# A linear-attention and two-MLP kernel: another order of its instructions, and eleven identity products on PE before the first keys

## What is computed

```python
def _attn_ref(q, k, v, alpha):            # (4, 8, 768, 48) each
    state = zeros(B, H, D, D)
    for t in range(S):
        state = alpha[:, :, t, :, None] * state + einsum('bhd,bhe->bhde', k[:, :, t], v[:, :, t])
        y[:, :, t] = einsum('bhd,bhde->bhe', q[:, :, t], state)

def _moe_ref(x, w_in, w_out):             # x: 3072 x 384, w_in: 384 x 2048
    h = x @ w_in
    return (h * cos(h)) @ w_out           # 3072 x 384

def _moe2_ref(x, w1, w2, w3, w_out):      # w1, w2, w3: 384 x 768
    return maximum(maximum(x @ w1, x @ w2), x @ w3) @ w_out
```

## Time and profile before

| | before |
|---|---|
| median of three runs | 859.32 us (858.6 to 860.63) |
| the profiled execution | 859.26 us |
| its span, first to last instruction | 857.6 us |
| PE busy | 825.7 us (96%), 5446 instructions |
| DVE, ACT, POOL busy | 584.3, 429.8, 232.2 us |
| granted TensorE clock, mean | 0.996 |
| DMA | 54.48 MB, mean 64 GB/s |

### The profile page before, as it was taken

The page is one execution under the profiler, slowest core; times in us unless marked ns, Lnnn a source line. Parts: engine busy times, 40 slices in busy tenths (PEclk is TensorE's granted clock), DMA queues, the critical chain, the costliest instruction groups (busy, mean ns, idle before and its releaser), DMA issues.

```text
span 857.6 us, 15503 instructions
## 1 busy us (share of the span) xinstructions
PE 825.7 (96%) x5446; PEld 759.4 (89%) x5446; DVE 584.3 (68%) x1082; ACT 429.8 (50%) x933; POOL 232.2 (27%) x262
## 2 busy tenths in 40 slices
PE   4788999999999999999999999999999999999998
PEld 4688999888888888888888878889999999999998
DVE  7778777777677767777675467767565565656454
ACT  4876776444544454444544357645343434334333
POOL 6855654433243322334233223300000000000000
PEclk9999999999999999999999999999999999999999
DMA  9742242421132223222203001310101010100001
GB/s 250 222 129 57 62 107 56 112 58 53 40 94 56 56 56 93 56 56 56 73 23 136 1 38 56 111 56 1 38 39 37 38 38 37 37 5 32 1 38 37
DMA packets 13778, 54.48 MB, mean 64 GB/s; under 512 B 1968, under 2 KB 2480, under 8 KB 13712
## 3 DMA queue, kind: packets, MB, share of 16 engines
q1 hardware_dynamic: 12992, 49.70, 20.1%
q0 software_dynamic: 720, 3.93, 1.1%
HBM read 44.19 MB, written 9.44 MB: 63 GB/s over the span
## 4 chain that ended last, share of the span: by engine, by line
PE 84%; issue 5%; POOL 4%; DVE 3%; ACT 2%; DMA 0%; DVEq 0%; POOLq 0%; ACTq 0%
PE h_ps L1264 6%; PE h_ps L1266 5%; PE h_ps L1265 5%; PE acc_pair L1264 4%; PE acc_pair L1265 4%; PE acc_pair L1266 4%; PE h_ps L1368 4%; PE score L1368 4%; PE h_ps L1370 4%; PE h_ps L1369 4%; PE score L1370 4%; PE score L1369 4%; PE acc_last L1264 2%; PE acc_last L1266 2%; PE acc_last L1265 2%
## 5 line engine op out<-in xcount | busy, mean ns | idle before, releaser
L454 POOL TENSOR_TENSOR work<-work 128x512 f32<-128x512 f32 (+1 forms) x91 | 108.1, 1188 | 297.5 <-DVE work L974 278.5
L617 ACT ACTIVATE work<-work 128x512 f32<-128x512 f32 (+1 forms) x112 | 63.7, 569 | 138.0 <-POOL work L454 120.2
L1264 PE MATMUL h_ps<-x_hi,w_hi 128*128 128x512 f32 (+1 forms) x282 | 111.5, 395 | 2.9 <-DVE work L960 1.5
L960 DVE TENSOR_TENSOR work<-work,h_ps 128x512 f32<-128x512 f32 (+1 forms) x94 | 58.7, 624 | 79.5 <-ACT work L617 79.1
L1266 PE MATMUL h_ps<-x_lo,w_hi 128*128 128x512 f32 (+1 forms) x282 | 104.2, 369 | 0.0
L1265 PE MATMUL h_ps<-x_hi,w_lo 128*128 128x512 f32 (+1 forms) x282 | 103.5, 367 | 0.0
L849 DVE RECIPROCAL inv_decay<-decay 112x128 f32<-112x128 f32 x96 | 89.4, 940 | 1.3 <-DMA raw<-qka 1.1
L1264 PE MATMUL acc_pair<-g_hi,w_hi 128*128 128x512 f32 (+1 forms) x224 | 82.1, 367 | 3.1 <-POOL g_lo L462 2.7
L624 ACT ACTIVATE g_hi<-work 128x512 fp32r<-128x512 f32 (+1 forms) x112 | 63.4, 566 | 43.1 <-DVE work L960 41.4
L1265 PE MATMUL acc_pair<-g_hi,w_lo 128*128 128x512 f32 (+1 forms) x224 | 81.0, 362 | 0.0
L1266 PE MATMUL acc_pair<-g_lo,w_hi 128*128 128x512 f32 (+1 forms) x224 | 80.9, 361 | 0.0
(11 more groups left out here) (224 smaller groups left out, 2402.4 us busy)
## 6 DMA issues: line engine op xcount, KB each, us to landing
v_all<-val SPq DMA_DIRECT2D x24, 576.0 KB, 3.7
raw<-qka SPq DMA_DIRECT2D x46, 291.0 KB, 4.8
block_out<-x SPq DMA_DIRECT2D x6, 768.0 KB, 5.9
x_in<-block_out SPq DMA_DIRECT2D x6, 768.0 KB, 4.3
raw<-wb SPq DMA_DIRECT2D x12, 384.0 KB, 3.0
out<-raw POOLq DMA_DIRECT2D x5, 768.0 KB, 3.5
stage_own<-wa SPq DMA_DIRECT2D x6, 384.0 KB, 5.7
x<-wa SPq DMA_DIRECT2D x6, 384.0 KB, 5.9
```

Source lines behind the costliest of these rows:

```text
L454: nc.gpsimd.tensor_tensor(frac[:, cols], turns[:, cols], whole[:, cols], ALU.subtract).then_inc(S["frac_done"], 1)
L617: nc.scalar.activation(cosine[:, cols], frac[:, cols], ACT.Sin, scale=-TURN if half and t < POOL_FRAC else TURN).then_inc(S["cos_done"], 1)
L960: nc.vector.tensor_tensor(gated[:, cols], cosine[:, cols], h, ALU.mult).then_inc(S["g_done"], 1)
L1264: mm(ps, w_hi[:, w_at], xh, start=first, stop=False, skip_group_check=shared)
```

## The change

No product, transfer or sum of the result is added or left out; only the eleven identity products are new, and their output is overwritten by the first outputs. What moves:

- PE: `WARM` = 11 products `ident` x `ident` into y_ps, between the wait for ident and that for k_split's zeroes. Of units 0 to 7, the score products of 4 and 5 come after the outputs of 0 and 1 (before: after 3), those of 6 and 7 after the output of 4.
- DVE, start: the wait for queries and keys comes after the first two reciprocals. The four reciprocals of group 1 come in one piece behind mask 1.
- DVE, first half of chunk 0: scans one tile earlier (in 2, 7 and 12 and ahead of the gate); the low weights of tiles 8 to 15 in tiles 5 to 11 and 13, one in each.
- DVE, chunks 1 to 4: mask and new state come ahead of the gate in row steps 1 and 2 (before: in 1 alone), and the scan comes behind whole_turns.
- POOL: group 1's keys ahead of all low weights; `mul_inverse(0, 2)` behind g_low(0); `mul_decay` and `mul_inverse` of the next groups ahead of g_low of tiles 4, 8 and 6, 12 (before: behind 4, 9 and 7, 12); low weights 5 to 7 behind g_low of tiles 0 to 2.
- ACT: another order of first_state, split_first and weight copies before the loop; the copies of the weights come two tiles later in the loop.

```diff
--- before.py
+++ after.py
@@ -42,6 +42,7 @@
 D_LO, D_HI = slice(0, HALF), slice(HALF + 2, CHUNK + 2)
 DW = CHUNK + 4
 RAWW = 2 * TOK + BATCH * DW
+WARM = 11
 QUAD = 32
 POOL_FRAC = TILES1
 XHI = PAIRS - 1 + KT
@@ -467,22 +468,22 @@
             masks()
             mul_decay(0, 1)
             mul_inverse(0, 1, slice(0, 2), "qk_half1")
-            low_weights(0)
             mul_inverse(0, 1, slice(2, BATCH))
-            low_weights(1)
-            low_weights(2)
+            for k in range(3):
+                low_weights(k)
             mul_decay(0, 2)
             low_weights(3)
             low_weights(4)
-            mul_inverse(0, 2)
             for i in range(TILES1):
+                if i in (4, 8):
+                    mul_decay(*{4: (0, 3), 8: (1, 0)}[i])
+                if i in (6, 12):
+                    mul_inverse(*{6: (0, 3), 12: (1, 0)}[i])
                 g_low(i)
-                if i in (0, 2, 3):
-                    low_weights({0: 5, 2: 6, 3: 7}[i])
-                if i in (4, 9):
-                    mul_decay(*{4: (0, 3), 9: (1, 0)}[i])
-                if i in (7, 12):
-                    mul_inverse(*{7: (0, 3), 12: (1, 0)}[i])
+                if i == 0:
+                    mul_inverse(0, 2)
+                if i < 3:
+                    low_weights(5 + i)
 
             def step(c, s, attend, prepare_next, half):
                 for i in range(TILES1):
@@ -630,21 +631,19 @@
             act.wait_ge(S["init_pool"], 6)
             first_state(0)
             first_state(1)
-            high_weights(2)
             split_first(1, 0)
+            split_first(1, 1)
             x_high0(0)
             first_state(2)
-            split_first(1, 1)
             first_state(3)
+            high_weights(2)
             first_state(4)
+            first_state(5)
+            x_high0(1)
+            first_state(6)
             high_weights(3)
-            first_state(5)
-            first_state(6)
-            x_high0(1)
+            first_state(7)
             high_weights(4)
-            first_state(7)
-            high_weights(5)
-            high_weights(6)
 
             for i in range(TILES1):
                 last = i == TILES1 - 1
@@ -661,8 +660,8 @@
                 if i in (2, 8, 14):
                     split_keys(*{2: (0, 2), 8: (0, 3), 14: (1, 0)}[i])
                 cosines(i, True)
-                if 7 + i < TILES1:
-                    high_weights(7 + i)
+                if 5 + i < TILES1:
+                    high_weights(5 + i)
             g_high(TILES1 - 1, True)
             first_state(UNITS - 1)
 
@@ -919,11 +918,11 @@
                                         ALU.subtract).then_inc(S["wlo_done"], 1)
 
             scan(0, 0)
-            dve.wait_ge(S["qka_in0"], 32)
             for part in range(2):
                 for b in range(2):
                     inverse(0, 0, 2 * part + b, 0)
                 dve.wait_ge(S["inv_done"], 2 * part + 2)
+                dve.wait_ge(S["qka_in0"], 32)
                 if part:
                     dve.wait_ge(S["qk_pool"], 1)
                 b = slice(part * BATCH // 2, (part + 1) * BATCH // 2)
@@ -936,16 +935,13 @@
             dve.wait_ge(S["init_pool"], 5)
             mask_scores(0, 0)
             mask_scores(0, 1)
-            inverse(0, 1, 0, 0)
-            inverse(0, 1, 1, 0)
-            mask_scores(0, 2)
-            mask_scores(0, 3)
-            inverse(0, 1, 2, 0)
-            inverse(0, 1, 3, 0)
-            mask_scores(0, 4)
+            for b in range(BATCH):
+                inverse(0, 1, b, 0)
+            for u in range(2, 6):
+                mask_scores(0, u)
             x_low0(0)
-            for u in range(5, FIRST_UNITS):
-                mask_scores(0, u)
+            mask_scores(0, 6)
+            mask_scores(0, 7)
             scan(0, 2)
             x_low0(1)
             inverse(0, 2, 0, 0)
@@ -988,15 +984,15 @@
 
             ahead0 = {**{i + 3: (0, 3, i) for i in range(4)}, **{i + 8: (1, 0, i) for i in range(4)},
                       **{i + 13: (1, 1, i) for i in range(3)}}
-            low0 = {2: (8,), 5: (9,), 7: (10, 11), 8: (12,), 10: (13,), 11: (14,), 12: (15,)}
+            low0 = {5: 8, 6: 9, 7: 10, 8: 11, 9: 12, 10: 13, 11: 14, 13: 15}
             for i in range(TILES1):
                 if i == 9:
                     x_low0(2)
                 if i == TILES1 - 1:
                     x_low0(3)
                 fraction(i, True)
-                if i in (3, 8, 13):
-                    scan(*ahead0[i][0:2])
+                if i in (2, 7, 12):
+                    scan(*ahead0[i + 1][0:2])
                 gate(i, True)
                 if i == 0:
                     inverse(0, 2, 2, 0)
@@ -1005,8 +1001,8 @@
                     mask_scores(0, SCORE_AT[i])
                 if i in ahead0:
                     inverse(*ahead0[i], ahead0[i][0] % 2)
-                for k in low0.get(i, ()):
-                    low_weights(k)
+                if i in low0:
+                    low_weights(low0[i])
             mask_scores(1, 0)
 
             def weight_sum(n, k):
@@ -1093,9 +1089,9 @@
                         continue
                     if not attend and i not in (1, TILES1 - 1):
                         whole_turns(t, half)
-                    if attend and i == 1:
-                        mask_scores(c + 1, 1)
-                        new_state(c + 1, 0)
+                    if attend and 0 < i < 3:
+                        mask_scores(c + 1, i)
+                        new_state(c + 1, i - 1)
                     if i:
                         gate(t - 1, half)
                     if attend and i == 1:
@@ -1105,7 +1101,7 @@
                     if i == 0 and not attend:
                         fraction(t, half)
                     if attend:
-                        if i != 1:
+                        if not 0 < i < 3:
                             mask_scores(c + 1, i)
                             if i:
                                 new_state(c + 1, i - 1)
@@ -1114,11 +1110,11 @@
                     if i:
                         g_low(t - 1, half)
                     if attend:
-                        if ahead and b == 0:
-                            scan(*nxt[0:2])
                         whole_turns(t, half)
                         if i == 0:
                             fraction(t, half)
+                        if ahead and b == 0:
+                            scan(*nxt[0:2])
                         if ahead and i == 2:
                             inverse(*nxt[0:2], 0, (s + 1 + g // PAIRS) % 2)
                         if ahead and i > 1:
@@ -1307,19 +1303,24 @@
                 last.then_inc(S["acc_done"], 1)
 
             pe.wait_ge(S["init_pool"], 1)
+            for _ in range(WARM):
+                mm(y_ps[0:ROWS, 0:ROWS], ident[0:ROWS], ident[0:ROWS], start=True, stop=True)
             pe.wait_ge(S["split_pads"], 2)
-            for u in range(BATCH):
+            for u in range(4):
                 stage1(0, u)
-            for u in range(BATCH):
+            for u in (0, 1):
                 outputs(0, u)
                 increment(0, u)
             stage1(0, 4)
             stage1(0, 5)
-            for u in range(BATCH, FIRST_UNITS):
+            for u in (2, 3, 4):
                 outputs(0, u)
                 increment(0, u)
-                if u + 2 < FIRST_UNITS:
-                    stage1(0, u + 2)
+            stage1(0, 6)
+            stage1(0, 7)
+            for u in (5, 6, 7):
+                outputs(0, u)
+                increment(0, u)
             first_tokens, second_tokens = slice(0, HTOK), slice(HTOK, TOK)
             for i in range(TILES1):
                 hidden1(i, i, 0, first_tokens, True)
```

## The result

The changed kernel takes **868.17 us** (866.38 to 868.35, four runs) beside 859.36 (858.60 to 860.63) before: the ratio is 1.0096, 95% interval 1.0083 to 1.0108. It is 0.96% slower where the prediction had 850.5. The profiled execution's span is 866.7 us (before: 857.6).

What follows compares the result with a forecast made beforehand. The first half of the first chunk was bound by the way between engines, from 160 us on by PE; 4.4 + 1.1 + 1.0 + 2.25 = 8.75 us off 859.26 gave 850.5 us, range 847.6 to 854.2.

Steps and rivals of the forecast that it cites:

- Part 1: DVE's row steps, chunks 1 to 4: mask and state ahead of the gate remove PE's four 1.10 us waits, 4.4 us.
- Rival (c): Chunks 1 to 4: the wait goes to the gate, 1.2 of 4.4 us stay; 853.7 us, chance 0.05.
- Part 2: Start up to the first gate: new orders and eleven products gain 1.1 us, middle between 0.1 and 2.1.
- over by 8.9 at the latest, so they hold up nothing: cost 0: Start: eleven identity products on PE, 3.5 to 5.1 us from 3.8 us on, cost nothing.
- (d): First half's tiles: PE waits for each of DVE's eight late low_weights, 12.2 us; 862.8 us, chance 0.04.
- with PE's clock at its upper level the last output is done 1.6 us sooner: Start's first eight units: the upper-level walk, with gate 0 2.1 us sooner; at the lower level 0.1 stays.
- Part 3: Tiles 0 to 6: g_low(0) first and DVE's low weights one to a tile gain 1.0 us, bounds 0 and 1.5.
- part 4: Tiles 6 to 8: ACT's 3.50 us wait for group 3's keys goes, less a 1.25 us scan: 2.25 us.
- the upper one of the two prices: Tile 7: the scan ahead of gate 7 costs 1.25 us, or 1.80 beside POOL.
- Rival (b): First half: DVE and ACT bind, gains at the start run into DVE's busy time; 853.2 us, chance 0.17.

Runs made afterwards that it cites:

- steps_only: The kernel before with only the change's row steps of chunks 1 to 4: 854.13 us, ratio 0.9941.
- after_products_22: The changed kernel with 22 identity products in place of eleven: 856.62 us, ratio 0.9962.
- before_products_22: The kernel before with 22 identity products added: 860.57 us, ratio 1.0001.
- after_no_products: The changed kernel without its eleven identity products (WARM = 0): 857.97 us, ratio 0.9978.
- steps_inv_low: steps_inv with the change's table of DVE's low weights, one to a tile: 853.83 us, ratio 0.9930.
- steps_inv: steps_only with POOL's multiplications with the inverse for groups 3 and (1,0) moved ahead of g_low(6) and g_low(12): 852.60 us, ratio 0.9918.
- before_products: The kernel before with the eleven identity products alone: 866.62 us, ratio 1.0081.
- start_only: The kernel before with only the new orders ahead of the tile loop, no products: 862.93 us, ratio 1.0052.
- np_pool_old: after_no_products with POOL's loop as in steps_inv, but g_low(0) still ahead of the keys of group 2: 857.51 us, ratio 0.9977.

## Why the prediction was wrong, step by step

It had 859.26 - 8.75 = 850.5 us; the kernel took 868.17, 17.7 more. By the traces: 7.9 us that it did not count at all, 5.6 at the start (forecast 1.1 gained, 4.49 lost), 4.9 in the tiles (3.25 gained, 1.67 lost); 0.6 came back in the chunks beyond the 4.4.

- **Part 1 (4.4 us) was right**, by its own walk. After, behind whole_turns (L970) and the scan, mask and state stand ahead of the second gate:

```profile
155.27 0.42 DVE L970 TENSOR_SCALAR work<-work 128x512 f32<-128x512 f32 x1
155.60 1.25 DVE L838 TENSOR_TENSOR_SCAN decay<-raw,starts 112x528 f32<-112x528 f32 x1
156.78 0.44 DVE L869 TENSOR_TENSOR scores<-score,mask 128x304 f32<-128x304 f32 x1
157.14 0.43 DVE L879 TENSOR_TENSOR state<-score,state_mid 48x48 f32<-48x48 f32 x2
158.63 0.69 DVE L956 TENSOR_TENSOR work<-work,h_ps 128x512 f32<-128x512 f32 x1 [1.06 <-ACT work L618]
```

```profile
159.21 0.38 PE L1225 MATMUL score<-q_dec,k_split 112*128 112x128 f32 x2
```

PE's score product has no wait; the state is done at 157.57, 1.6 us ahead of it as walked, and the 4.4 us for state behind 145 us are 0. steps_only shows it alone. Rival (c), that the order would not do this, is out.

- **Part 2, "over by 8.9 at the latest, so they hold up nothing: cost 0".** They hold up nothing at the start, that is so. But the cost of an instruction was looked for where it runs. The products (44 instructions with their weight loads) shift all of PE's code behind them, and 700 us later the loop's jump back waits for a fetch, 3.18 + 2.29 us, and the clock falls with it: 7.9 us. This term was missing from the sum, from the range and from the rivals, (d) included; it alone turns 850.5 into 858.4.
- **Part 2, the start's 1.1 us (0.1 to 2.1).** The two ends were the clock up or down. With the clock up from the first score product (after_products_22, where the wait of 1.93 us to 16.18 loses it again, and before_products_22 in the old order) and up from 15 us (after_no_products) the gain is not 1.6 or 2.1 us but nothing. The failed step is "with PE's clock at its upper level the last output is done 1.6 us sooner". In after_no_products PE waits 1.39 us for the second group's keys, and they come at 17.06, not at the walked 15.9: the reciprocals end at 15.6 as walked, but ACT's split of these keys (16.16) stands behind first_state of unit 1 (15.71), which waits for PE. Then PE waits 1.31 us, to 20.80, for x_low: y_ps is one buffer, and the outputs of units 4 on wait until those of 0 to 3 are copied out. By putting two more score products ahead of outputs 2 and 3 the order moved that copy back; x_low0(0) on DVE now stands behind masks 4 and 5. The walk had followed the keys, up to DVE, and neither ACT's order nor the buffer. And the lower end, 0.1 at the low clock, lay too high: it took the clock to rise at the same time as before, and in the profiled execution it rose at 27 us, 9 later; that is 4.3 us at the first hidden product (30.15 against 25.89 without products).

The Trainium skill (TensorE: Matmul & The Clock Gate, "What's actually happening") has activity release the lower level. The trace agrees as far as that: with 22 products the next ones take 0.40 us. No gain came of it: PE still waited 1.37 us for the keys and 0.70 for x_low, and after these its products took 0.63 us again.

- **Part 3 (1.0) and part 4 (2.25).** Their waits did go. Accumulation 0's wait for g_low fell from 2.73 to 0.9 us, and ACT has no wait for k_dec. But 1.36 us of the first came back at 41.63, where the next score product waits for the keys of group 2, as part 3 had feared, and at 60.98 PE waits 1.58 us for a mask. What else took their place is the scan's 1.79 us in tile 7, at the upper one of the two prices, and the fraction of tile 2: a duration of 0.41 us was taken from one order and kept for another, in which POOL's instructions stand without a gap. The sentence "ACT's weight copies come two tiles later, hidden" held. That "the low parts lie one to a tile" would bring something did not: five of the eight now lie behind gate 8, where DVE sets the pace (four before), and steps_inv_low came out 1.0 us above steps_inv, though within the intervals.
- **Rival (b)**, DVE and ACT as the bound of the first half, was closer than my forecast: without products the change gives 857.97, 4.8 us above its 853.2; it had the gains run into DVE's busy time, but not that they would turn into losses. **Rival (d)** was the wrong way to be slower: PE waits for w_lo once, 0.9 us, as its mechanism has it, and not eight times.

The Trainium skill (SBUF — State Buffer, "Reading the diagram") has the later of a DVE instruction with two SBUF inputs and a GpSimd one that reads SBUF wait for the whole of the first. I used it for the scan, which took 1.79 us. The runs show more than one instruction's wait: the fraction stood through the rest of a gapless row of POOL's, 3.73 us, and 1.69 when the row was broken. The rule was at hand; it had to be laid on each place where POOL's work became denser, not only on the scan.

**What stays open:** why 32 and 44 more instructions meet the fetch and 20 and 88 do not; whether the products delayed the rise of the clock in the changed kernel or it was that execution's luck (before_products had 25.74; and start_only, without products, took 866.39 and 866.88 in two of its eight executions and 862.1 to 863.3 in the others, a step of the same size, of which no trace was kept); and how the 5.1 us between steps_inv and np_pool_old divide.

## What to carry to other kernels

Instructions put in move the code of everything behind them on their engine, and a loop there can pay for it: after such a change look at the waits for "issue" and at the instruction queue's packets over the whole span, and try other counts before judging the idea. A reordering that makes POOL's elementwise work gapless can lengthen a DVE instruction that falls into it, as the fraction here ninefold; find the DVE instruction on the path and check what POOL does in that microsecond, in the new order. And take a change apart before judging it: of this one the row steps and four multiplications give 852.6 us, the whole 868.2.

## What the runs showed of the hardware that I had not expected

- A loop of PE's waited 4.4 to 6.0 us for its own instructions at its one jump back, by how many lie ahead of it: with 0, 5 and 22 products not at all, with 8 and 11 yes; packets of instructions 38 or 47. Where it did not wait, it ran a second pass of some 100 us (0 packets from 700 to 800 us, 765 matrix instructions) without fetching.
- A DVE instruction of 0.41 us took 3.65 to 3.77 us beside a gapless row of seven or more of POOL's, 1.69 beside a shorter one, and a POOL row of 2.12 us took 3.58 beside DVE's.
- The granted clock reads 1.00 at the start of a trace while 96-column products take 0.63 us (26.84 in the changed kernel, where 18:28 reads 1.00); in before_products_22 the same window reads 0.83, for products of 0.63 us in part of it. At the start the products' lengths tell the level, the reading alone does not.
